# Weight splits of the mix stage: six chunks in attention instead of ten, four in the first pair of the mix

## The reference, cut to what matters

```python
# 1. attention in chunks of 32 queries, 8 heads of 64, over 8 memory keys and 56 neighbours
scores = scale * np.matmul(q_c, k_full.transpose(0, 1, 3, 2))
a = np.exp(scores - max); a = a / (a.sum + 1e-09)
out[:, :, c_start:c_end] = np.matmul(a, v_full)
# 2. the mix: xk and xr are blends of a token with the token before it
k = np.maximum(xk @ w_k, 0.0)            # "up", 512 -> 1024
v = k * k @ w_v                          # "down", 1024 -> 512
r = 1.0 / (1.0 + np.exp(-(xr @ w_r)))    # "gate", 512 -> 512
x2 = r * v
# 3. every token goes to one of 8 experts (a sticky choice along the sequence)
out = p[e] * (np.maximum(x2 @ w1[e], 0.0) @ w2[e])
```

## Time and profile before

| | us |
|---|---|
| median of 3 runs (498.55 to 500.6) | 498.62 |
| the profiled execution's own time | 499.68 |
| its span, first to last instruction | 498.0 |
| PE busy | 446.9 (90%) |
| DVE busy | 262.7 (53%) |
| ACT busy | 222.1 (45%) |
| POOL busy | 52.9 (11%) |
| mean granted PE clock, as a share of full speed | 0.948 |

### The profile page before, as it was taken

How to read it: one execution, slowest core, us unless ns; L and a number is a source line. 1 busy time by engine, 2 the same in 40 slices (tenths; PEclk the granted TensorE clock), 3 DMA queues, 4 the chain that set the end, 5 groups by cost and what they waited for, 6 DMA issues and landing times.

```text
span 498.0 us, 9958 instructions
## 1 busy us (share of the span) xinstructions
PE 446.9 (90%) x3792; PEld 371.4 (75%) x3792; DVE 262.7 (53%) x592; ACT 222.1 (45%) x332; POOL 52.9 (11%) x70
## 2 busy tenths in 40 slices
PE   2775759999999999999999779999999999999991
PEld 2654549898898988988987557777777777777771
DVE  3576883434745447465584618223732274646851
ACT  2445652723537345372571036223712373727740
POOL 0001000000100101001001211111100011112110
PEclk9987578999999999999999879999999999999997
DMA  8889649753090540901901486410751176575610
GB/s 319 336 289 395 243 156 386 293 205 135 8 372 5 214 167 20 360 0 42 356 5 44 149 333 196 170 41 22 231 169 42 44 215 207 185 227 160 237 29 11
DMA packets 23728, 87.34 MB, mean 175 GB/s; under 512 B 3150, under 2 KB 3278, under 8 KB 23696
## 3 DMA queue, kind: packets, MB, share of 16 engines
q1 hardware_dynamic: 18048, 70.87, 39.1%
q0 software_dynamic: 5360, 16.04, 9.4%
q10 hardware_dynamic: 288, 0.02, 0.0%
HBM read 55.34 MB, written 32.62 MB: 177 GB/s over the span
## 4 chain that ended last, share of the span: by engine, by line
PE 72%; DMA 11%; DVE 7%; issue 5%; ACT 2%; POOLq 1%; POOL 0%; DVEq 0%; SPq 0%; ACTq 0%
PE PS L607 15%; PE PS L463 14%; PE PS L496 13%; PE PS L590 13%; PE PS L479 7%; DMA XR<-expert_rows 6%; PE PS L598 2%; PE PS L517 2%; PE PS L575 2%; DMA RAW<-wmix 2%; DMA QK<-tiles 1%; DMA VV<-tiles 1%; DVE EL L1084 1%; PE PS L507 1%; ACT WHI L703 1%
## 5 line engine op out<-in xcount | busy, mean ns | idle before, releaser
L1084 DVE TENSOR_TENSOR EL<-ERAW,EH 128x1024 fp32r<-128x1024 f32 x56 | 66.5, 1218 | 2.8 <-DVE META L1159 2.7
L781 ACT ACTIVATE EH<-ERAW 128x1024 fp32r<-128x1024 f32 x56 | 57.5, 1055 | 8.8 <-PE PS L607 8.8
L1152 DVE TENSOR_TENSOR HL<-PS,HH 128x512 fp32r<-128x512 f32 x32 | 22.1, 691 | 68.3 <-ACT HH L795 68.3
L607 PE MATMUL PS<-EH,HH 128*128 128x512 f32 x128 | 55.0, 430 | 3.3 <-issue 0.9
L463 PE MATMUL PS<-XHI,WHI 128*128 128x256 f32 x192 | 56.7, 295 | 0.9 <-issue 0.9
L590 PE MATMUL PS<-EH,XSH 128*128 128x512 f32 x128 | 53.3, 417 | 3.6 <-DVE EL L1084 3.6
L463 PE MATMUL PS<-XHI,WLO 128*128 128x256 f32 x192 | 55.2, 288 | 0.0
L463 PE MATMUL PS<-XLO,WHI 128*128 128x256 f32 x192 | 55.1, 287 | 0.0
L590 PE MATMUL PS<-EH,XSL 128*128 128x512 f32 x128 | 51.5, 402 | 0.0
L590 PE MATMUL PS<-EL,XSH 128*128 128x512 f32 x128 | 51.4, 402 | 0.0
L607 PE MATMUL PS<-EH,HL 128*128 128x512 f32 x128 | 50.9, 398 | 0.0
(11 more groups left out here) (147 smaller groups left out, 814.9 us busy)
## 6 DMA issues: line engine op xcount, KB each, us to landing
ERAW<-wexp SPq DMA_DIRECT2D x56, 512.0 KB, 5.0
expert_rows<-ZR SPq DMA_DIRECT2D x6, 4112.0 KB, 13.8
QK<-tiles SPq DMA_DIRECT2D x12, 768.0 KB, 6.4
VV<-tiles SPq DMA_DIRECT2D x12, 520.0 KB, 6.2
RAW<-wmix POOLq DMA_DIRECT2D x10, 512.0 KB, 6.0
XR<-expert_rows POOLq DMA_DIRECT2D x17, 257.0 KB, 4.5
CO<-consts SPq DMA_DIRECT2D x1, 340.0 KB, 4.8
rows_out<-OSB,OIDX POOLq DMA_INDIRECT x16, 5.3
```

The costliest lines, as they stand in the source:

```text
L607: last = nc.tensor.matmul(PS[4][:, :], x[:, f, :], ww[:, c:c + D], start=n == 0, stop=n == 23)
L781: nc.scalar.activation(expert_part(EH1, EH2, w, c), ERAW[c][:], ACT.Copy).then_inc(ehi_done, 1)
L1084: nc.vector.tensor_tensor(expert_part(EL1, EL2, w, c), ERAW[c][:], expert_part(EH1, EH2, w, c).bitcast(F32), ALU.subtract).then_inc(elo_do ...
L1152: nc.vector.tensor_tensor(HL[:, 4 * part:4 * part + 4, :].rearrange("p k n -> p (k n)"), PS[2 + part][:, :], HH[:, 4 * part:4 * part + 4, ...
```

## The change

Attention now splits only chunks 0 to 5, at t = 2, 3, 4, 5, 8 and 9. Chunks 4 and 5 move from t = 6 and 7 to t = 8 and 9, where chunks 6 and 7 were. Chunks 6 to 9 are split in the first pair of the mix, one behind each group q on ACT and on DVE. POOL's load of chunk 6 waits in addition for the product with V of tile 9 (`pv_done` 10).

```diff
--- before.py
+++ after.py
@@ -52,6 +52,8 @@
 XTW = NT * P + B
 C_ID, C_LT, C_ONE, C_REV, C_THR, C_TOK = 0, 128, 256, 384, 400, 496
 C_NF, C_POS, C_EXP, C_SLOT, CW = 508, 520, 584, 648, 808
+
+CHUNK_AT = {2: 0, 3: 1, 4: 2, 5: 3, 8: 4, 9: 5}
 
 SLAB = 52800
 FRESH_AT = -1.5 * 2.0 ** -23
@@ -710,8 +712,8 @@
                     x_out(t - 1)
                 if t + 2 < NT:
                     exps(t + 2, u, False)
-                if t >= 2:
-                    weight_hi(t - 2)
+                if t in CHUNK_AT:
+                    weight_hi(CHUNK_AT[t])
                 if t in (6, 7):
                     mix_scaled(0, t - 6, True)
                 if t in (8, 9):
@@ -799,10 +801,14 @@
                 if not first:
                     x2_out(2 * g - 2, 0)
                 relu_square(g, 0, first)
-                if not first:
+                if first:
+                    weight_hi(len(CHUNK_AT))
+                else:
                     x2_out(2 * g - 1, 1)
                 for q in range(1, 4):
                     relu_square(g, q, first)
+                    if first:
+                        weight_hi(len(CHUNK_AT) + q)
                     if last and q == 2:
                         for j in range(NPAIR):
                             act.wait_ge(xg_init[j], 16)
@@ -949,8 +955,8 @@
                 if t + 2 < NT:
                     shifted(t + 2, u, False)
                 normed(t, u, t < 2)
-                if t >= 2:
-                    weight_lo(t - 2)
+                if t in CHUNK_AT:
+                    weight_lo(CHUNK_AT[t])
                 if t in (6, 7):
                     mix_full(0, t - 6, True)
                 if t in (8, 9):
@@ -1099,20 +1105,27 @@
 
                 p = g - 1
                 squared(g, 0, first)
-                if not first:
+                if first:
+                    weight_lo(len(CHUNK_AT))
+                else:
                     logits_out(2 * p)
                 if last:
                     first_expert()
                 squared(g, 1, first)
-                if not first:
+                if first:
+                    weight_lo(len(CHUNK_AT) + 1)
+                else:
                     logits_out(2 * p + 1)
                 squared(g, 2, first)
                 if first:
+                    weight_lo(len(CHUNK_AT) + 2)
                     dve.wait_ge(tables_in, 16)
                     nc.vector.tensor_scalar(PRE[:, 1, :], eights, float(CAP // P), None, ALU.mult)
                 else:
                     flags(p)
                 squared(g, 3, first)
+                if first:
+                    weight_lo(len(CHUNK_AT) + 3)
                 lo(0)
                 lo(1)
                 lo(2)
@@ -1286,6 +1299,8 @@
                     pool.wait_ge(wlo_done, n - 1)
                 else:
                     pool.wait_ge(scores_done, n + 2)
+                if n == len(CHUNK_AT):
+                    pool.wait_ge(pv_done, NT - 2)
                 pool.dma_start(RAW[n % 2][:], wmix[:, n * CH1:(n + 1) * CH1]).then_inc(raw_loaded[n % 2], 16)
 
             def x_load(row):
```

## The result

The changed kernel took 496.41 us in the median of 10 executions (492.13 to 498.1), the kernel before 499.74 us (497.35 to 501.28, 10 executions). The ratio is 0.9931, 95% interval 0.9903 to 0.996. That is 3.3 us less, where 1.9 us were forecast from 498.62 us; the forecast of 496.7 us lies 0.3 us from the measured median, but part of that is chance, since the median before came out 1.1 us higher than in the three runs shown first. The interval of this first ratio stands for 2.0 to 4.8 us, so it just leaves the forecast's 1.9 us out; that of e5 holds it. All executions together, 110 of the kernel before with a mean of 498.95 us and 22 of the changed kernel with 496.33 us, give 2.6 us, within some 0.9 us either way.

What follows compares the result with a forecast made beforehand. Attention tiles 6 and 7 were taken as bound by ACT and DVE, with PE carrying the chain afterwards. Their 1.90 us, all other terms 0, took 498.62 to 496.7 us; own range 496.1 to 497.4, all runs 494.2 to 498.9 us.

Steps and rivals of the forecast that it cites:

- Tiles 6 and 7, 0.95 us each: Attention tiles 6 and 7: losing WHI and WLO moves XF up by ACT's 0.95 us each, 1.90 us together.
- Tiles 8 and 9 at 0: Attention tiles 8 and 9: they keep a WHI and a WLO, now of chunks 4 and 5; nothing changes, 0.
- the ladder: Tiles 6 and 7 bound by ACT and DVE in turn: PR, WHI, XF on ACT, then XF and MX on DVE.
- Tiles 10 and 11 at 0: End of attention: removed WHI and WLO worth 0, since the next instructions on ACT and DVE already waited.
- The loads at 0: Weight loads beside attention: four fewer, but no engine of tiles 6 and 7 waits for a transfer, so 0.
- The first pair at 0: First pair of the mix: load 8 lands in 3.9 us, last KLO 2.5 us ahead of down, cost 0.
- rival (b): First pair: load 8 late, costing its landing less 6.4 us; at 8.28 us, 498.6 us in all. Chance 0.08.
- The zero-fill: Starts near 92 instead of 74.3 us, each transfer still landing ahead of the scatter needing it; cost 0.
- rival (c): Late zero-fill holds up small transfers: FL queues, PE stands 6.5 us before its ranks, 503.2 us. Chance 0.04.
- The clock: PE's slow clock costs 1.35 us at up's start and 1.2 us in the last tiles; the sum leaves it.
- rival (a): PE's clock rises in last tiles and up: 2.55 us more off, 494.2 us. Chance 0.25; against, 497.8 us, 0.08.

Runs made afterwards that it cites:

- e5: The changed kernel again with no edit, measured beside the kernel before: 497.48 us against 499.58 us, ratio 0.9948.
- e1: Changed kernel, but chunks 6 and 7 split in tiles 10 and 11, so only tiles 6 and 7 are freed: 497.34 us against 498.91 us before.
- e2: Changed kernel, but splits at t = 2 to 9 as before, only tiles 10 and 11 freed: 499.17 us against 498.91 us before.
- e9: Changed kernel with chunks 4 and 5 moved to tiles 10 and 11, so tiles 6 to 9 have no split: 494.13 us against 499.09 us before.
- e4: Changed kernel with the zero-fill waiting for the end of attention, so beside loads 8 and 9: 502.21 us against 498.91 us before.
- e6: Changed kernel plus ten spare matmuls on PE at the end of attention: 495.6 us against 499.58 us before.
- e8: Changed kernel without POOL's added wait for tile 9's product with V: 496.15 us against 499.58 us before.
- e11: Changed kernel with tiles 6 to 9 unsplit, ten spare matmuls ending attention, 34 more ahead of the first expert's second slot: 495.32 us against 499.09 us before.
- e12: The kernel before against itself, no edit: 499.38 us against 499.46 us, ratio 1.0023.

## Why the prediction was right

*Tiles 6 and 7, 0.95 us each.* Right in place and size. The profile after shows 5.41 and 5.42 us; freeing these two tiles alone gives the gain (e1), and freeing the other two alone does not (e2). The choice of ACT's 0.95 over DVE's 1.23 us was right too: DVE's extra wait is in the trace.

*Tiles 8 and 9 at 0.* Right, tile 8 stayed at 5.46 us. They were not free of the ladder, though: e9 takes 1.06 us out of tile 8.

*Tiles 10 and 11 at 0.* Right by e2.

*The loads at 0.* Right as read, wrong as a rule for all executions. In e2 the split of tile 6 waited 0.57 us for its load and the tile took 0.68 us more. The changed kernel uses chunk 4 two tiles later, and none of its three profiles lost this. It may be a part of what lies between the 1.9 us of the sum and the 2.1 and 3.3 us measured; no run separates it, and the intervals of e1 and e5 hold 1.9 us. That the forecast of 496.7 us came within 0.3 us of the median is therefore partly luck.

*The first pair at 0.* Right: landings of 4.0 and 3.9 us, the last KLO ended at 88.3 us, 2.5 us ahead of down, which is the slack that the prediction reckoned. The point at which rival (b) begins to cost held in e4 within 0.4 us. What it left out is the clock: a wait of 2.5 us cost 4.4 us.

*The zero-fill, rival (c).* Loads 8 and 9 had the transfers to themselves. FL was late as feared, but little: beside the third zero-fill, issued at 102.4 us, it landed 6.3 us after issue instead of 1.9, and DVE stood 4.8 us for it. The ranks at 129.41 us came 2.49 us earlier than in the earlier trace rows, as all else did. The small transfer did not queue behind the large one, which landed 1.7 us after it, at 124.2 us.

*The clock, rival (a).* It did not turn up by itself: up began slow after (12.91 us) as before. The clock did rise in tiles 6 and 7, to 0.68 and 0.99, where it gives nothing, and was back at 0.50 in tile 8. Its price at up's start was right: 1.35 us reckoned, 1.31 measured in e6. Its price in the last tiles was 0.4 us for each of three groups, 1.2 us in all. The price of one group holds. PE has five on the path there, three of transposes and two products with V, and the stretch took 12.03 us with three of them slow (before and after), 12.40 us with four (e2) and 12.86 us with all five (e5, e8, at a clock of 0.50). No profile has all five fast, so whether the last 1.2 us can be had stays open. One and the same kernel differs by 0.8 us here between two executions (after and e5), and the rows that are longer are PE's slow ones. By the Trainium skill (TensorE: Matmul & The Clock Gate, "Part 1: The HAM clock gate") activity releases the throttle; e6 agrees at up's start, where ten more matmuls that do no work made 12.91 into 11.60 us.

## What to carry to other kernels

When two engines pass work to and fro in each step, an instruction taken off both is worth its time on the one whose next product the other waits for, not the larger of the two; look for the row that would start next and for what it would then wait. Work can be moved for nothing to where each next instruction on its engine already waits (here tiles 10 and 11, and the up stage), but a load that moves along must not meet a large transfer there: a hidden load that is late costs its wait and then, as in e4, slow matmuls as well. A change of 0.4% is hard to see in medians: ten or twelve executions gave intervals of 0.3% either way here, and one kernel's median came out at 2.1 and at 3.3 us of gain. The stage's own windows tell it sooner.

## What the runs showed of the hardware

- A wait of 2.5 us of PE within dense matmuls was followed by a granted clock of 0.74, then 0.50, then 0.62 over the next 4.5 us (e4), though PE was busy again all the time. The lower level came after the wait was over.
- Loads 8 and 9, 512 KB each and issued by POOL, took 4.0 and 3.9 us with no large transfer beside them and 9.3 and 9.1 us in e4 beside two zero-fills of 4112 KB issued by SP. Load 8 was there at 91.75 us, 7.9 us ahead of the second zero-fill, which was issued 9 us before it: the transfers of the two engines share. The two zero-fills, both from SP and 0.4 us apart, do not look like sharing: they landed after 14.0 and 23.9 us (after), and one alone took 12.3 us (the third before), so the second mostly came behind the first.
- Two later groups of matmuls, each behind a wait of PE, run fast in some profiles and slow in others. In the first expert's second slot the first 18 took 6.2 to 7.0 us in ten of the fourteen profiles and 4.46 us in four (e1, e2, e4, e11). In the last pair of the mix up's second 24 took 4.46 us in five (before, after, e5, e8, e11) and 2.94 us in nine, e12 among them, which is the kernel before. Together that is up to 4 us of the some 6 us over which executions of one kernel scatter; what decides the level stays open.

```profile
233.97 4.46 PE PS L463 x24
```

(the chain of the kernel before) and

```profile
234.41 2.94 PE PS L463 x24
```

(the same kernel in e12).
